# Contiguous left operands, unguarded scatters, a filler product, and a later request for a weight matrix in a fused attention and mixture-of-experts kernel

## What is computed

```
# soft mixture: phi 512x32, w1 8x512x1024, w2 8x1024x512
logits = x @ phi
d = softmax(logits over rows);  slot_input = (d.T @ x)            # per expert 4 slots
h = maximum(slot_input[e] @ w1[e], 0);  slot_out[e] = h @ w2[e]
x = softmax(logits over slots) @ slot_out
# switch mixture: expert_emb 8x512, w1 8x512x1024, w2 8x1024x512
logits = normalise(x) @ normalise(expert_emb).T / tau
expert_idx = argmax(logits);  gate_w = softmax(logits)[expert_idx]
for e in experts: out[rows of e] = gate_w * (maximum(x[rows] @ w1[e], 0) @ w2[e])
```

## Time and profile before

| | us |
|---|---|
| median of 3 executions | 369.28 |
| lowest, highest | 368.68, 370.42 |
| the profiled execution | 368.98 |
| its span in the trace | 367.3 |
| TensorE busy | 324.2 (88% of the span) |
| VectorE, ScalarE, GpSimd busy | 175.8, 143.3, 100.8 |

### The profile page before, as it was taken

How to read it: one execution, slowest core, us unless ns; L and a number is a source line. 1 busy time by engine, 2 the same in 40 slices (tenths; PEclk the granted TensorE clock), 3 DMA queues, 4 the chain that set the end, 5 groups by cost and what they waited for, 6 DMA issues and landing times.

```text
span 367.3 us, 8979 instructions
## 1 busy us (share of the span) xinstructions
PE 324.2 (88%) x3264; PEld 233.9 (64%) x3265; DVE 175.8 (48%) x406; ACT 143.3 (39%) x329; POOL 100.8 (27%) x181
## 2 busy tenths in 40 slices
PE   1879979989988999999977599999999999999991
PEld 0566657666766773433427158888888888888880
DVE  2577768777786552550214678323232223313231
ACT  1466667676787432131110073322223131313231
POOL 5566656666676000000000000122121211112121
PEclk9999999999999999899996999999999999999997
DMA  7999999999999907989950930021111101010110
GB/s 306 356 424 411 421 424 425 419 422 418 419 419 408 396 7 261 416 343 435 369 237 0 344 117 1 30 78 46 47 42 43 57 29 57 29 57 29 57 60 31
DMA packets 15147, 81.64 MB, mean 222 GB/s; under 512 B 2312, under 2 KB 2312, under 8 KB 10512
## 3 DMA queue, kind: packets, MB, share of 16 engines
q1 hardware_dynamic: 11936, 73.08, 49.1%
q0 software_dynamic: 1920, 6.29, 4.5%
q10 hardware_dynamic: 1264, 1.92, 1.6%
HBM read 74.99 MB, written 6.29 MB: 221 GB/s over the span
## 4 chain that ended last, share of the span: by engine, by line
PE 60%; DMA 19%; DVE 6%; ACT 5%; POOL 4%; issue 3%; SPq 2%; DVEq 0%; ACTq 0%; POOLq 0%
PE ps L918 34%; DMA ring<-in_vt 11%; DMA ring<-in_moe_w 8%; PE ps L638 3%; POOL ring L511 3%; PE ps L651 3%; PE ps L904 3%; PE ps L608 3%; ACT work L985 2%; PE ps L756 2%; DVE ps L1171 2%; PE ps L805 2%; PE ps L659 2%; PE ps L717 1%; PE ps L936 1%
## 5 line engine op out<-in xcount | busy, mean ns | idle before, releaser
L918 PE MATMUL ps<-high_w2b,hid_high 128*128 (+1 forms) x184 | 71.7, 390 | 0.0
L918 PE MATMUL ps<-low_w2b,hid_high 128*128 (+1 forms) x184 | 71.7, 390 | 0.0
L918 PE MATMUL ps<-high_w2b,hid_low 128*128 (+1 forms) x184 | 71.6, 389 | 0.0
L985 ACT ACTIVATE work<-ps,small 128x120 f32<-128x120 f32 x192 | 53.9, 368 | 38.9 <-DVE small L1175 38.6
L564 POOL DMA_INDIRECT out_x<-work,small x24 | 23.6, 982 | 143.4 <-DVE small L1408 88.2
L1415 DVE SCALAR_TENSOR_TENSOR hid_low<-ps,hid_high 128x1024 fp32r<-128x1024 f32 x26 | 31.8, 1224 | 56.6 <-ACT hid_high L1086 56.5
L1068 ACT ACTIVATE work<-ps,small 128x512 f32<-128x512 f32 x24 | 16.5, 690 | 94.0 <-PE ps L918 87.3
L608 PE MATMUL ps<-ident,work 128*120 128x128 f32 x192 | 32.2, 292 | 10.8 <-ACT work L985 10.6
L918 PEld LDWEIGHTS ps<-high_w2b,hid_low 128*128 128x128 f32 x184 | 34.5, 188 | 7.3
L918 PEld LDWEIGHTS ps<-high_w2b,hid_high 128*128 128x128 f32 x184 | 34.6, 188 | 6.9
L918 PEld LDWEIGHTS ps<-low_w2b,hid_high 128*128 128x128 f32 x184 | 34.6, 188 | 6.7
(11 more groups left out here) (230 smaller groups left out, 366.3 us busy)
## 6 DMA issues: line engine op xcount, KB each, us to landing
ring<-in_moe_w SPq DMA_DIRECT2D x12, 2048.0 KB, 11.9
ring<-in_qk SPq DMA_DIRECT2D x16, 1104.0 KB, 14.2
ring<-in_v SPq DMA_DIRECT2D x16, 780.0 KB, 10.2
ring<-in_moe_w SPq DMA_DIRECT2D x10, 512.0 KB, 17.9
x_or_g<-in_moe_w SPq DMA_DIRECT2D x2, 2048.0 KB, 10.1
ring<-in_vt SPq DMA_DIRECT2D x7, 384.0 KB, 8.9
comb<-in_vt SPq DMA_DIRECT2D x7, 384.0 KB, 8.5
whole_w2b<-in_moe_w SPq DMA_DIRECT2D x4, 512.0 KB, 9.1
```

The source lines that it names most:

```text
L918: last = pe.matmul(ps[:, 4 + u, :], hidden_part[:, u, m * P:(m + 1) * P], matrix[:, bass.ds(e * UNIT + m * DM, DM)], start=m == 0 and i == ...
L985: last = act.activation(probs[u][:, j, :], sc[u][:, j // 2, (j % 2) * KC:(j % 2 + 1) * KC], ACT.Exp, bias=negmax[u][:, j:j + 1], scale=flo ...
```

## The change

There are four parts.

1. The copy to `si_sb` and the ReLU to `h_sb` now read PSUM in steps of four elements and write four contiguous groups of 128 columns. TensorE takes contiguous left operands in both places. The halves of `si_sb` are now column groups, so L734's first two products wait for the first half alone.
2. GpSimd no longer waits for a scatter's rows to land. ScalarE and VectorE wait on `rows_out[u]` themselves, and not at all for the first item. SP waits for all of them at the end of its program (`all_written`). `many_head` belongs to a branch that doesn't run with these inputs.
3. One matmul whose result nobody reads stands between the two halves of the last down product.
4. SP waits for piece 0 of the up matrix (`w1b_part[0]`) before it requests the down matrix.

```diff
@@ -254,7 +254,7 @@
         cpart_ready = sem("cpart_ready"); cT_done = sem("cT_done"); cT_ready_a = sem("cT_ready_a"); cT_ready_d = sem("cT_ready_d")
         hid_done = sem("hid_done"); hid_ready_a = sem("hid_ready_a"); hid_ready_d = sem("hid_ready_d")
         y_tile_done = sem("y_tile_done"); o_ready = [sem(f"o_ready{u}") for u in range(2)]; id_ready = sem("id_ready")
-        scatter_issued = sem("scatter_issued"); rows_left = sem("rows_left"); rows_out = [sem(f"rows_out{u}") for u in range(2)]
+        scatter_issued = sem("scatter_issued"); all_written = sem("all_written"); rows_out = [sem(f"rows_out{u}") for u in range(2)]
 
         def unit_of(kidx):
 
@@ -280,9 +280,13 @@
             eng.dma_start(unit_of(kidx).rearrange("p (f r) -> p f r", f=halves),
                           t[e].rearrange("(f p c) n -> p f (c n)", f=halves, p=P)).then_inc(unit_loaded[kidx], 16)
 
-        def every_fourth(rows, c):
-
-            return rows.rearrange("p (q c) -> p c q", c=DC)[:, c, :]
+        def by_fours(rows):
+
+            return rows.rearrange("p (q c) -> p c q", c=DC)
+
+        def column_groups(rows):
+
+            return rows.rearrange("p (c q) -> p c q", c=DC)
 
         def load_last(eng, half, u):
             t, e = units[2 * E - 2 + u]
@@ -428,6 +432,7 @@
                     .then_inc(w1b_part[c], 16)
             n_used = load_experts(sp)
             with sp.If(n_used < FEW + 1):
+                sp.wait_ge(w1b_part[0], 16)
                 for c in range(4):
                     rows = slice(2 * c * P, 2 * (c + 1) * P)
                     sp.dma_start(whole_w2b[:, 0, c * UNIT // 4:(c + 1) * UNIT // 4].rearrange("p (c n) -> p c n", n=DM),
@@ -446,6 +451,11 @@
                     for r in range(E):
                         with sp.If(n_used > r):
                             load_matrix(w2b, r, unit_of(r), w2b_loaded)
+            sp.wait_ge(list_ready, 1)
+            n_items = sp.value_load(items_i[0:1, 3 * LIST + E + 1:3 * LIST + E + 2], min_val=NPT, max_val=NIT)
+            for u in range(2):
+                sp.wait_ge(rows_out[u], n_items * 16)
+                sp.sem_inc(all_written, 1)
 
 
         @block.gpsimd
@@ -458,7 +468,6 @@
                 ins.then_inc(pool_seq, 1)
                 pool.wait_ge(pool_seq, seq[0])
 
-            pool.sem_inc(rows_left, 2)
             pool.memset(mask[:, :, :], 0.0)
             pool.memset(band, 0.0)
             pool.memset(vb[0], 0.0)
@@ -563,8 +572,6 @@
                 pool.sem_inc(scatter_issued, 1)
                 pool.indirect_dma_start(out, bass.IndirectOffsetOnAxis(id_buf[u], 0), o_sb[u], None,
                                         bounds_check=NTOK - 1, oob_is_err=False).then_inc(rows_out[u], 16)
-                pool.wait_ge(rows_out[u], n * 16 + 16)
-                pool.sem_inc(rows_left, 1)
 
             pool.wait_ge(list_ready, 1)
 
@@ -729,9 +736,9 @@
 
             pe.wait_ge(selr_ready, 1)
             for c in range(DC):
-                if c == 0:
-                    pe.wait_ge(si_ready, 2)
-                last = pe.matmul(ps[:, 1, c * SLOTS:(c + 1) * SLOTS], every_fourth(si_sb, c), selr,
+                if c % 2 == 0:
+                    pe.wait_ge(si_ready, c // 2 + 1)
+                last = pe.matmul(ps[:, 1, c * SLOTS:(c + 1) * SLOTS], si_sb[:, c * P:(c + 1) * P], selr,
                                  start=True, stop=True)
             last.then_inc(siT_done, 1)
 
@@ -786,7 +793,7 @@
                     pe.wait_ge(combT_ready, 1)
                 pe.wait_ge(h_ready, pr + 1)
                 for m in range(4):
-                    last = pe.transpose(ps[:, 2 + pr % 2, m * P:(m + 1) * P], every_fourth(h_sb[pr % 2], m),
+                    last = pe.transpose(ps[:, 2 + pr % 2, m * P:(m + 1) * P], h_sb[pr % 2][:, m * P:(m + 1) * P],
                                         ident[:, :])
                 last.then_inc(hT_done, 1)
                 if pr == 2:
@@ -799,6 +806,8 @@
                     pe.wait_ge(unit_loaded[4 * pr + 3], 16)
                 for m in range(4):
                     if pr == E // 2 - 1 and m % 2 == 0:
+                        if m:
+                            keep_at_work(1, 1, comb[:, 0:BANK // SLOTS, :].rearrange("p q s -> p (q s)"))
                         for u in range(2):
                             pe.wait_ge(last_half[m // 2][u], 32)
                     for j in range(4):
@@ -1017,8 +1026,9 @@
             act.activation(L_sb, flat[:, 4 * BANK:4 * BANK + S], ACT.Copy).then_inc(l_ready, 1)
             act.wait_ge(si_done, 1)
             for u in range(2):
-                half = slice(u * DM // 2, (u + 1) * DM // 2)
-                act.activation(si_sb[:, half], ps[:, 0, half], ACT.Copy).then_inc(si_ready, 1)
+                half = slice(u * DC // 2, (u + 1) * DC // 2)
+                act.activation(column_groups(si_sb)[:, half, :], by_fours(ps[:, 0, :])[:, half, :], ACT.Copy)\
+                   .then_inc(si_ready, 1)
             act.wait_ge(cexp_in, 1)
             act.activation(comb[:, :, :], comb[:, :, :], ACT.Exp).then_inc(cexp_done, 1)
 
@@ -1026,7 +1036,8 @@
                 act.wait_ge(h_done, pr + 1)
                 if pr >= 2:
                     act.wait_ge(hT_done, pr - 1)
-                act.activation(h_sb[pr % 2], ps[:, pr % 2, :], ACT.Relu, scale=rowmask[:, pr:pr + 1])\
+                act.activation(column_groups(h_sb[pr % 2]), by_fours(ps[:, pr % 2, :]), ACT.Relu,
+                               scale=rowmask[:, pr:pr + 1])\
                    .then_inc(h_ready, 1)
                 if pr == 1:
                     act.wait_ge(emb_squares, 1)
@@ -1064,7 +1075,8 @@
 
             def gated(n, u, q2):
                 act.wait_ge(y_tile_done, n * 2 + u + 1)
-                act.wait_ge(rows_left, n * 2 + u + 1)
+                if not (isinstance(n, int) and n == 0):
+                    act.wait_ge(rows_out[u], n * 16)
                 act.activation(o_sb[u], ps[:, 4 + u, :], ACT.Copy, scale=gates[:, bass.ds(q2 * 2 + u, 1)])\
                    .then_inc(o_ready[u], 1)
 
@@ -1404,7 +1416,8 @@
                 dve.tensor_copy(g_stage[:, :], g_flat[:, bass.ds(e * F, F)]).then_inc(g_staged, 1)
 
             def ids(n, u, code):
-                dve.wait_ge(rows_left, n * 2 + u + 1)
+                if not (isinstance(n, int) and n == 0):
+                    dve.wait_ge(rows_out[u], n * 16)
                 dve.tensor_copy(id_buf[u], ids_u[:, bass.ds(code * 2 + u, 1)]).then_inc(id_ready, 1)
 
             def hidden_of(u):
@@ -1486,6 +1499,9 @@
             link(dve.tensor_tensor(ids_v, ids_v, row_no.unsqueeze(1).broadcast_to([P, E, NQ]), ALU.add))
             link(dve.tensor_copy(ids_u, ids_f))
 
+            def many_head():
+                one_item(second_half)(0)
+
             def few_head():
                 code = look_up(dve, 2, 0)
                 stage(2, (hid_done, 2))
@@ -1497,7 +1513,7 @@
             with dve.If(n_used < FEW + 1):
                 each_item(dve, one_item(low_part), few_head)
             with dve.If(n_used > FEW):
-                each_item(dve, one_item(second_half))
+                each_item(dve, one_item(second_half), many_head)
 
 
 _INS = ["moe_phi", "moe_w1", "moe_w2", "moe2_expert_emb", "moe2_tau", "moe2_w1", "moe2_w2"]
```

## The result

| | before | changed |
|---|---|---|
| median, us (executions) | 368.99 (4) | 364.40 (4) |
| lowest, highest | 368.68, 370.42 | 364.18, 365.16 |
| ratio [95% interval] | | 0.989 [0.985, 0.993] |
| the profiled execution | 368.98 | 364.45 |

The changed kernel is 4.6 us faster at the median. Measured again it took 364.75 us (6 executions) beside 368.39 (19), ratio 0.990 [0.987, 0.993]. Over the 61 executions of before that were measured beside the experiments the mean is 368.3 us (from 366.4 to 371.3 us), and over all ten of the changed kernel it is 364.65. So the change is worth **3.7 us**, and the 4.6 us hold some 0.9 us of chance: the first four executions of before have a mean of 369.3 us.

A forecast was written before the change was run, and what follows sets the result against it. TensorE's own work was taken to bound the switch stage, leaving the stretch ahead of it and the end: 368.98 - 2.2 (end) - 0 (operands) - 0 (filler) - 0 (requests) = 366.8 us, range 365.2 to 369.3 us.

The forecast's parts named there:

- Operands: Ahead of the switch stage: contiguous left operands save TensorE time, but the last weights' landing stays; 0 us, bounds 0 and 0.9.
- the last weights land sooner: Rival at the last down product: a different DMA engine is late, so the earlier request helps; 365.6 us, chance 0.15.
- the 0.9 us that the prediction named: Request of units 10 and 11, at 156.29 us when the first up product is done, goes out 0.9 us sooner.
- The reads of PSUM in steps of four: ScalarE's strided PSUM reads cost 0 to 0.7 us on ScalarE and 0 on the path, covered by the wait.
- The end: After the last matmul: GpSimd's DRAIN runs beside the last scatter's landing; gain 2.2 us, bounds 0 and 2.4.
- The filler: Extra product in TensorE's idle time before the last half unit lands: takes 592 ns, costs 0 us.
- the slower rival: Clock falls at the last down product after longer idling, doubling products there: +3.1 us, 369.9 us, chance 0.13.
- The requests: Chosen expert's matrices: requesting the down matrix behind the up matrix gains 0, at most 0.3 us; cost 0, at most 0.8.
- The 2.3 us of room for the down matrix: Down matrix's last piece lands at about 215.6 us and is read at 217.9, so a later request costs 0.

The follow-up runs named there:

- the two kernels with three fillers: Changed kernel with three fillers ahead of the last halves and one in each of five short gaps; the second adds three before the up matrix; medians 364.90 and 364.66 us.
- part 1 alone: Kernel before with only the contiguous left operands for the slot inputs and the ReLU output; median 366.93 us, ratio 0.997.
- changed, no filler: Changed kernel without the matmul between the two halves of the last down product; median 365.06 us, ratio 0.991.
- changed, GpSimd waits: Changed kernel with GpSimd waiting once for all landings after its loop, ahead of its DRAIN; its span ends at 364.6 us.
- changed, again: Changed kernel measured once more, unaltered, for its spread and a second profile; 364.75 us, ratio 0.990.
- changed, late DRAIN: Changed kernel with GpSimd waiting for all landings at the end, then making 12 memsets before its DRAIN; two executions, 366.36 and 369.36 us.
- part 2 alone: Kernel before with only GpSimd's waits for the scatters' landings removed and SP waiting at its end; median 367.76 us, ratio 0.999.
- before, again: Kernel before, unaltered, in a second profiled execution; 369.58 us.
- part 3 alone: Kernel before with only one product added between the halves of the last down product; median 367.57 us, ratio 0.9995.
- changed, slot inputs strided: Changed kernel with the slot-input products' left operands strided again and the ReLU output contiguous; median 366.68 us, ratio to before 0.994.
- part 4 alone: Kernel before with only the down matrix requested after piece 0 of the up matrix has landed; median 368.55 us, ratio 1.001.
- fillers throughout: Changed kernel with three fillers ahead of the last halves, one in each of five gaps and five in the up matrix's wait; median 364.66 us, ratio 0.991.

## Why the prediction was right in direction and too small

**Operands: the term that failed.** The prediction set it to 0, between 0 and 0.9 us. Its step was that the landing at 190.9 us stays, since the late DMA engine at 190 us would be the same as the one at 156 us and have no idle time to lose. The landing follows the request instead, and 12 profiled executions size it (the two kernels with three fillers are left out, since theirs don't wait). The times are the request of units 10 and 11 and the start of the second half, by the trace's clock and then from the end of the logits. That end differs between executions, and it is read from the single request that goes out right behind the logits, as in these rows of before and of the changed kernel:

```profile
138.31 0.38 SPq L280 DMA_DIRECT2D ring<-in_moe_w  x1
...
138.96 0.38 SPq L280 DMA_DIRECT2D ring<-in_moe_w  x1
```

| kernel | request | second half | request, from the logits | second half, from the logits |
|---|---|---|---|---|
| part 1 alone | 153.40 | 188.55 | 15.04 | 50.19 |
| changed, no filler | 153.47 | 188.85 | 15.03 | 50.41 |
| changed, GpSimd waits | 153.58 | 188.60 | 15.04 | 50.06 |
| changed, again | 153.94 | 189.03 | 15.03 | 50.12 |
| changed | 154.00 | 189.04 | 15.04 | 50.08 |
| changed, late DRAIN | 154.02 | 189.29 | 15.04 | 50.31 |
| part 2 alone | 154.77 | 190.16 | 16.28 | 51.67 |
| before, again | 154.79 | 190.44 | 16.29 | 51.94 |
| part 3 alone | 154.88 | 189.77 | 16.29 | 51.18 |
| changed, slot inputs strided | 155.46 | 190.47 | 16.29 | 51.30 |
| part 4 alone | 156.26 | 190.68 | 17.98 | 52.40 |
| before | 156.29 | 191.00 | 17.98 | 52.69 |

Counted from the logits the requests fall into three groups. With contiguous slot inputs the request comes after 15.0 us and the second half after 50.2 (six executions, 50.06 to 50.41). With strided ones and no fall of the clock near 151 us it is 16.3 and 51.5 (four, 51.18 to 51.94). With strided ones and that fall it is 18.0 and 52.5 (two). So the 1.25 us that the slot inputs bring to the request arrive whole, as 1.3 us, and of the 1.7 us that the fall costs the request 1.0 arrives. The pair that differs in the slot inputs alone (changed, and changed with strided slot inputs) gives 1.22 us for 1.25. A straight line through the times by the trace's clock has a slope of 0.81 us of landing for a us of request, and leaves 0.25 us; from the logits it is 0.83. The term of the operands thus measures 1.3 us, where the prediction had 0 and a bound of 0.9. Of the 1.96 us between the two first profiles it is the larger part. The rest is, roughly, those two executions: a fall in the one, for 1.0 us, and an attention that ended 0.65 us later in the other. That rest is luck, and no gain of the change.

The windows of the two first profiles (columns as in the earlier trace rows) show where the fall of the clock costs the DMA time. In before the DMA engines run dry around the request:

```profile
156.00:156.50 0.50, 0.50 (x12) 0.15 (x8) 0.47 (x2) 0.20 (x1) 0.00 (x0) 1.00 0.24 98
```

In the changed kernel the request comes while most of them are at work:

```profile
154.00:154.50 0.50, 0.50 (x8) 0.13 (x4) 0.47 (x2) 0.49 (x1) 0.00 (x0) 1.00 0.61 262
154.50:155.00 0.50, 0.50 (x8) 0.13 (x4) 0.47 (x2) 0.19 (x1) 0.00 (x0) 1.00 1.07 459
```

A share of 0.24 leaves twelve of the 16 engines idle, and that is capacity lost. That two are late at 156 us and one at 190 us didn't show that it was the same one. The 1.25 us of the slot inputs can't be seen in the shares. They are seen in the bytes. These are the 46 us from the logits on, of before, of before again and of the changed kernel:

```profile
138.31:184.31 46.00, 42.99 (x335) 17.05 (x339) 15.63 (x36) 9.51 (x17) 0.00 (x0) 0.96 0.94 370
138.50:184.50 46.00, 42.72 (x343) 17.11 (x343) 15.63 (x36) 10.30 (x19) 0.00 (x0) 1.00 0.97 380
138.96:184.96 46.00, 42.40 (x355) 16.69 (x359) 16.44 (x38) 10.67 (x19) 0.00 (x0) 1.00 0.97 390
```

The share is 0.97 in both of the last two, but they moved 380 and 390 GB/s. Over 46 us that is 0.46 MB, which at the 431 GB/s of the earlier trace rows takes 1.1 us, near the 1.3 us of the landing. Which engine is late at the end, and why, stays open, since the rows don't tell the engines apart. The rival "the last weights land sooner" was this mechanism, with a chance of 0.15 and 365.6 us.

The request itself moved further than the 0.9 us that the prediction named, by 2.29 us between the two first profiles. Three things make it up. The products take 1.02 us less (2.02 to 1.00), and the first of them start 0.2 us sooner, since they wait for one half of `si_sb` alone: 1.25 us together, measured from the end of the logits. Against it, attention ended 0.65 us later in that execution. The remaining 1.7 us are the clock. In the profiled execution of before it was at 0.50 from 151.5 us, and from the start of the first up product to the request it took 5.4 us (150.89 to 156.29). In the changed kernel it took 3.7 us (150.30 to 154.00), and in the second execution of before 3.7 us too (151.09 to 154.79). The prediction had this fall before it and took the request time of that one execution for the kernel's own. Two of the six profiles with strided slot inputs have the fall near 151 us and none of the eight with contiguous ones, which is too few to say whether the change prevents it.

The reads of PSUM in steps of four, for which it had bounds of 0 and 0.7 us on ScalarE, cost nothing at all. Line 1039 of the changed kernel takes what L1029 took the earlier trace rows:

```profile
L1039 ACT ACTIVATE work<-ps,rowmask x4: 687/687/689, 154.0 to 182.6; 128x512 f32<-128x512 f32 x4
```

The Trainium skill, page "Advanced Engine Details and Errata", section "PSUM Cachelines", wants every two consecutive elements contiguous for the best throughput, and names matmuls as what gets slow otherwise. The prediction carried this over to ScalarE. This row, FP32 with a step of 16 bytes on ScalarE, doesn't agree with that.

**The end: right mechanism, term mis-sized.** 2.2 us were forecast and 1.39 measured (from the landing to the end of the span it was 2.65 us in all five profiles that have the old form, and 1.26 us in all seven with the new one). The DRAIN is a cost of its own, as said (late DRAIN, 2.04 us). But with the scatter in flight the DRAIN still ends 1.0 us behind the landing, where the prediction had all of it done before. That, and not the mechanism, is what the term had wrong. The bounds of 0 and 2.4 us held it. The Trainium skill's 12 ns for a DRAIN (page "VectorE: DVE Perf Modes") fits SP's 13 ns row and none of GpSimd's.

**The filler: 0, as forecast, but priced from half of it.** One product of FP32 is two records, 1.12 us, not the 592 ns of a single row. It still fits into the 2.2 us between the halves. What it does for the clock was told under the slower rival. Of the executions profiled with one filler, none of six had the clock down in the second half. Without it, three of the four that idled 2.2 us or more had it (2.20, 2.24 and 2.47 us; the fourth idled 2.34 us), and neither of the two that idled 1.2 to 1.5 us. So the rival's mechanism is seen, and the filler stands exactly where it would have struck. That the filler is what prevents it rests on ten traces. The two short ones had also had a fall at 151 us, so idling isn't all that differs. Its price was 3.1 us in the prediction, with both products doubled. In the three traces that have it the second half takes 1.1 to 1.5 us more (3.02, 3.06 and 3.46 us for 1.92), and in two of them L820's products another 0.75 (1.91 for 1.16), 1.5 to 1.9 us in all. What the filler brings on the average of executions is smaller, since not every one falls: 0.6 us alone on before and 0.8 us in the changed kernel (365.4 to 364.65), neither beyond its interval.

**The requests: 0, as forecast.** The 2.3 us of room for the down matrix hold, and the up matrix is not helped by an empty queue.

**The clock, a term that the sum didn't have.** Each execution lists its mean granted clock. From it comes the time at the lower level, span x (1 - mean) / 0.5. It includes the end of the span, behind the last matmul, where the lower level costs nothing (4.3 us in the first profile of before, 3.0 with fillers throughout). Its means are 15.0 us for before, 15.2, 16.0 and 15.3 with parts 1, 2 and 4 alone, 11.9 with the filler alone, 10.7 changed, 11.2 changed with strided slot inputs, 12.9 changed without the filler, 5.9 and 4.1 with more fillers. Over all executions, with a mean for each kernel, a microsecond more at the lower level goes with 0.30 us more time (+- 0.04). So 4.3 us less is worth 1.3 us. The pieces of the mean 3.7 us are then the end (1.4), the request through the landing (1.0 by the slope of 0.81, 1.3 by the groups) and the clock (1.3). They add up to 3.7 to 4.0 us. Part of the clock's piece belongs to the parts above, so this division is an estimate, and that it adds up proves nothing. That the clock's piece is caused by the filler isn't shown. It is a correlation, and the kernels with more fillers should have gained another 1.4 to 2.0 us by it and didn't.

## What to carry to other kernels

Follow a late landing back to its own request, and the request back to what releases it; a low DMA share just after a request is capacity lost, and one late engine is no argument against it unless the rows show the same engine in both places. Compare bytes moved as well as shares, and count from a common event when two executions are compared. Look at the closing DRAIN of the engine that ends last, and expect only part of it back when it can begin sooner. Ahead of a sum, take a second profile of the kernel before, since the places where the clock falls differ between executions, and here one of them put 1.7 us on the request's time.

## What the runs showed of the hardware

- GpSimd's DRAIN takes 2.03 us after all its work is done, 4 us after the last landing too, and ends 1.0 us after the landing of a scatter that is in flight when it begins.
- A strided left operand (FP32, a step of 16 bytes) is dear: eight products of 128x32 took 2.02 us with it and 1.00 us without. ScalarE's read of PSUM with the same step cost nothing (687 ns beside 689).
- Executions of one kernel, measured together on one core, differ by up to 4.8 us (before, 31 executions, 366.35 to 371.14 us), and the places where the granted clock falls differ with them. With fillers throughout, the six executions lay within 1.1 us (364.38 to 365.49).
